# Attention and two expert layers on one core: orders of ScalarE, PE and GpSimd at three joints, and T forms by input tiles

## The reference: what is computed

```python
attn = softmax(where(mask, q @ k.T / 8, -1e9)) @ v        # -> x [1152, 512]
h = np.maximum(x @ w_in, 0.0)                             # w_in [512, 2048]
x = h * h @ w_out                                         # w_out [2048, 512]
p = domain_probs / (domain_probs.sum(-1, keepdims=True) + 1e-09)
for e in range(4):                                        # w1[e] [512, 1024], w2[e] [1024, 512]
    h = np.maximum(x @ w1[e], 0.0)
    out += p[:, e:e + 1] * (h @ w2[e])
```

## Time and profile before

| | us |
|---|---|
| median of 3 runs (641.86 to 643.49) | 642.8 |
| the profiled execution | 641.86 |
| its span, first to last instruction | 640.1 |
| PE matmuls busy | 619.5 (97%) |
| DVE busy | 375.0 |
| POOL busy | 293.8 |
| ACT busy | 247.7 |

### The profile page before, as it was taken

One profiled execution on the slowest core, in us unless ns is written; L12 is line 12 of the kernel. 1 busy time (PEld: TensorE's weight loads), 2 busy tenths in 40 slices (PEclk: granted clock), 3 DMA queues, 4 the chain that ended last, 5 costly groups with the idle time before them and its releaser, 6 DMA issues.

```text
span 640.1 us, 11296 instructions
## 1 busy us (share of the span) xinstructions
PE 619.5 (97%) x4182; PEld 576.7 (90%) x4182; DVE 375.0 (59%) x980; ACT 247.7 (39%) x674; POOL 293.8 (46%) x249
## 2 busy tenths in 40 slices
PE   8879898999999999999999999999999999999998
PEld 7769897999999999989899899899899889889986
DVE  4876557585585586673564564564565465456452
ACT  6997655362362363461151151241241331232210
POOL 4987784255055058695065064074073173260200
PEclk9999998999999999999999999999999999999999
DMA  8440301012022012021011021011021022020012
GB/s 321 158 133 2 132 2 67 1 67 67 1 67 67 2 66 68 0 67 67 1 67 67 1 67 66 2 67 67 0 67 67 1 66 67 2 67 1 0 51 98
DMA packets 16486, 35.87 MB, mean 56 GB/s; under 512 B 2864, under 2 KB 3120, under 8 KB 16432
## 3 DMA queue, kind: packets, MB, share of 16 engines
q1 hardware_dynamic: 16432, 35.15, 16.4%
HBM read 32.79 MB, written 2.36 MB: 55 GB/s over the span
## 4 chain that ended last, share of the span: by engine, by line
PE 83%; DVE 7%; ACT 6%; issue 2%; POOL 2%; DVEq 0%; ACTq 0%; POOLq 0%
PE ps L1122 27%; PE ps L1124 26%; PE ps L1123 26%; ACT prob L548 3%; DVE h_lo L873 2%; DVE ps L860 1%; PE ps L1119 1%; DVE ps L866 1%; POOL xf_lo L482 1%; DVE prob L725 1%; PE ps L1065 1%; ACT xf_hi L595 1%; PE ps L1111 1%; ACT h_hi L622 1%; ACT wa_hi L572 1%
## 5 line engine op out<-in xcount | busy, mean ns | idle before, releaser
L1122 PE MATMUL ps<-xf_hi,wa_hi 128*128 128x288 f32 x672 | 200.4, 298 | 4.1 <-ACT m L608 3.7
L1123 PE MATMUL ps<-xf_lo,wa_hi 128*128 128x288 f32 x672 | 199.2, 296 | 0.0
L1124 PE MATMUL ps<-xf_hi,wa_lo 128*128 128x288 f32 x672 | 198.6, 296 | 0.0
L448 POOL TENSOR_TENSOR wb_lo<-raw_b,wb_hi 128x512 fp32r<-128x512 f32 x48 | 60.7, 1303 | 186.6 <-ACT wb_hi L581 186.6
L1122 PEld LDWEIGHTS ps<-xf_hi,wa_hi 128*128 128x128 f32 x672 | 127.0, 189 | 5.7 <-ACT wa_hi L572 3.5
L1123 PEld LDWEIGHTS ps<-xf_lo,wa_hi 128*128 128x128 f32 x672 | 126.9, 189 | 0.5
L1124 PEld LDWEIGHTS ps<-xf_hi,wa_lo 128*128 128x128 f32 x672 | 127.3, 189 | 0.0
L1122 PE MATMUL ps<-wb_hi,h_hi 128*128 128x512 f32 x288 | 112.3, 390 | 1.1 <-DVE h_lo L876 1.1
L1124 PE MATMUL ps<-wb_hi,h_lo 128*128 128x512 f32 x288 | 112.4, 390 | 0.0
L1123 PE MATMUL ps<-wb_lo,h_hi 128*128 128x512 f32 x288 | 112.4, 390 | 0.0
L903 DVE SCALAR_TENSOR_TENSOR y<-ps,p_norm,y 128x512 f32<-128x512 f32 (+1 forms) x64 | 47.4, 742 | 96.1 <-PE ps L1124 96.1
(11 more groups left out here) (77 smaller groups left out, 868.6 us busy)
## 6 DMA issues: line engine op xcount, KB each, us to landing
raw_a<-in_wa SPq DMA_DIRECT2D x48, 256.0 KB, 3.8
raw_b<-in_wb SPq DMA_DIRECT2D x24, 512.0 KB, 4.9
q_buf<-in_q SPq DMA_DIRECT2D x8, 288.0 KB, 4.7
k_buf<-in_k SPq DMA_DIRECT2D x8, 288.0 KB, 4.6
result<-y SPq DMA_DIRECT2D x8, 256.0 KB, 2.0
v_loc<-in_v_near SPq DMA_DIRECT2D x4, 384.0 KB, 4.6
v_str<-in_v_far SPq DMA_DIRECT2D x4, 320.0 KB, 5.5
result<-y SPq DMA_DIRECT2D x2, 128.0 KB, 1.8
```

The source lines that it names most:

```text
L448: nc.gpsimd.tensor_tensor(wb_lo[:, :, cols], raw_b[:, :, cols], wb_hi[:, :, cols].bitcast(F32), ALU.subtract).then_inc(s_wb_lo, 1)
L1122: nc.tensor.matmul(dst, a_hi, b_hi, start=first, stop=False)
L1123: nc.tensor.matmul(dst, a_hi, b_lo, start=False, stop=False)
L1124: return nc.tensor.matmul(dst, a_lo, b_hi, start=False, stop=last)
```

## The change

- Attention's end, ACT: `first_product(0)` and one `x_high` come ahead of `att_out(6)`. PE: unit 1 of M2 goes behind `outputs(6)` and the transposes of pair 7.
- Block 0: the squares of C22 and C12 are made by ACT (new `squared`, activation Square) and no longer by DVE; ACT's order of h_high, y_copy and x_high is another.
- Block 2: ACT's `first_product(2)` moves up between relu and h_high of block 1's C12.
- Parts B of blocks 1 to 6: DVE takes y tile 1 between the two units of h_low (C22) and c_block (C12) of the block that went ahead.
- Experts' entry: T2, T3 and T4 of sets 2 and 3 are made in halves of one input tile each (new `half_forms`), during the parts B of blocks 6 and 7. ACT's x_high(3, ...) are spread among the h_high of block 8. POOL makes wb_low of group 4 ahead of the sums of group 5.

The diff, cut to its core:

```diff
-            return {T1: 1, T2: 2, T3: 3, T4: 4}[k]
+            return {T1: 1, T2: 5, T3: 6, T4: 7}[k]
...
-                if kind == "A" and t % 2 == 0 and 0 < t and s + 1 < SUBS:
+                if kind == "A" and t % 2 == 0 and t not in (0, BLOCKS1) and s + 1 < SUBS:
                     sums(s + 1, S1, S3, S2, S4)
                 if kind == "A" and t % 2 == 1:
                     if t > 1:
                         for d in range(KT):
                             wb_low(s, d)
-                    if t == 1:
-                        sums(1, S1, S3, S2, S4)
+                    if t in (1, BLOCKS1 + 1):
+                        sums(s + 1, S1, S3, S2, S4)
...
+            def squared(t, q):
+                for u in range(2):
+                    act.wait_ge(s_relu, tile_count(t, q, u))
+                    nc.scalar.activation(ps[:, hbank(t, q, u), 0:HT], relu[:, u, :], ACT.Square).then_inc(s_sq, 1)
...
-            att_out(NP - 2)
             first_product(0)
             x_high(0, 3)
+            att_out(NP - 2)
...
             rectified(0, C22)
+            squared(0, C22)
+            h_high(0, C22)
             y_copy(0)
             x_high(1, 1)
-            h_high(0, C22)
+            rectified(0, C12)
+            squared(0, C12)
+            h_high(0, C12)
             y_copy(1)
-            rectified(0, C12)
             x_high(1, 2)
-            y_copy(2)
-            h_high(0, C12)
-            y_copy(3)
-            for k in (3, 4, 5, 6):
-                x_high(1, k)
-                y_copy(k + 1)
+            for k in (2, 3, 4, 5):
+                y_copy(k)
+                x_high(1, k + 1)
+            y_copy(6)
+            y_copy(7)
...
+                    if t == BLOCKS1 - 1:
+                        x_high(3, 0)
                     continue
-                first_product(t)
+                if t != 2:
+                    first_product(t)
                 if t == 1:
...
+                    rectified(1, C12)
+                    first_product(2)
+                    h_high(1, C12)
                     wa_high(1, 6)
                     continue
+                if t == BLOCKS1:
+                    x_high(3, 1)
+                    x_high(3, 2)
+                    h_high(t, C11)
+                    x_high(3, 3)
+                    h_high(t, C21)
+                    x_high(3, 4)
+                    x_high(3, 5)
+                    h_high(t, C22)
+                    x_high(3, 6)
+                    h_high(t, C12)
+                    continue
...
-                if t == BLOCKS1:
-                    for k in range(FORMS):
-                        x_high(3, k)
...
+            def half_forms(i, kt):
+                c = i % 2
+                blocks, b12 = x_blocks(c)
+                dve.wait_ge(s_y, y_tiles(BLOCKS1 - 4 + i) + KT + 2 * (kt + 1))
+                for k in (T2, T3, T4):
...
+                    nc.vector.tensor_tensor(t_form[:, c, k, kt, :], a[:, kt, :], b[:, kt, :], ALU.subtract)\
+                        .then_inc(s_t[i], 1)
...
-            for u in range(2):
-                square(0, C22, u)
...
-            for u in range(2):
-                square(0, C12, u)
...
-                    if t == BLOCKS1:
-                        t_forms(3, T3, T4)
...
-                            if i == 0:
-                                for u in range(2):
-                                    h_low(follows[1], C22, u)
-                                    c_block(follows[1], C12, u)
+                            if i < 2:
+                                h_low(follows[1], C22, i)
+                                c_block(follows[1], C12, i)
...
-                        if t == BLOCKS1 - 2 and i == KT - 1:
-                            t_forms(2, T1)
-                        if t == BLOCKS1 - 1 and i == 0:
-                            t_forms(2, T3)
-                        if t == BLOCKS1 - 1 and i == 1:
-                            t_forms(2, T4)
-                        if t == BLOCKS1 - 1 and i == KT - 1:
-                            t_forms(3, T1)
-                    if t >= BLOCKS1 - 2:
-                        t_forms(t - BLOCKS1 + 4, T2)
+                        if t >= BLOCKS1 - 2 and i == KT - 1:
+                            t_forms(t - BLOCKS1 + 4, T1)
+                        if t >= BLOCKS1 - 2 and i in (KT + 1, KT + 3):
+                            half_forms(t - BLOCKS1 + 4, (i - KT) // 2)
...
-                    product(0, M2)
+                    product(0, M2, [0])
...
             prob_transposes(NP - 1, 0)
+            product(0, M2, [1])
             product(0, M6, [0])
```

More of the change, by code:

```diff
@@ L681, in _ @@
                             x_high(2, k)
+                    if t == BLOCKS1 - 1:
+                        x_high(3, 0)
                     continue
-                first_product(t)
+                if t != 2:
+                    first_product(t)
                 if t == 1:
-                    for q in (C11, C21, C22, C12):
+                    for q in (C11, C21, C22):
                         rectified(1, q)
-                        if q != C12:
-                            wa_high(1, 2 * q)
+                        wa_high(1, 2 * q)
                         h_high(1, q)
-                        if q != C12:
-                            wa_high(1, 2 * q + 1)
+                        wa_high(1, 2 * q + 1)
+                    rectified(1, C12)
+                    first_product(2)
+                    h_high(1, C12)
                     wa_high(1, 6)
+                    continue
[10 more added lines that the diff above has]
+                    h_high(t, C12)
                     continue
@@ L758, in t_forms @@
                     else:
-                        dve.wait_ge(s_y, y_tiles(BLOCKS1 - 4 + i) + (KT if k == T1 else 2 * KT))
+                        dve.wait_ge(s_y, y_tiles(BLOCKS1 - 4 + i) + KT)
                     if k == T1:
@@ L770, in t_forms @@
                     nc.vector.tensor_tensor(t_form[:, c, k, :, :], a, b, ALU.subtract).then_inc(s_t[i], 1)
+            def half_forms(i, kt):
[3 more added lines that the diff above has]
+                for k in (T2, T3, T4):
+                    if k == T2:
+                        dve.wait_ge(s_t[i], 1)
+                        a, b = blocks[B22], t_form[:, c, T1, :, :]
+                    elif k == T3:
+                        a, b = blocks[B22], b12
+                    else:
+                        dve.wait_ge(s_t[i], 3 * kt + 2)
+                        a, b = blocks[B21], t_form[:, c, T2, :, :]
+                    nc.vector.tensor_tensor(t_form[:, c, k, kt, :], a[:, kt, :], b[:, kt, :], ALU.subtract)\
+                        .then_inc(s_t[i], 1)
             def pair_t1(n):
```

## The result

| | before | changed |
|---|---|---|
| median, us | 642.33 (4 runs, 641.78 to 643.49) | 637.66 (4 runs, 637.22 to 638.49) |
| ratio | | 0.9927, 95% interval 0.9908 to 0.9946 |
| profiled execution, its span | 641.86, 640.1 | 637.22, 635.4 |

The change makes the kernel 4.7 us faster (3.5 to 5.9 by the interval), where 8.0 us was forecast. The forecast was 634.8, range 632.8 to 637.5: right way, and too low by 2.9 us. A fourth run of the kernel before (641.78) moved its median from the 642.8 that the forecast started from to 642.33.

What follows compares the result with a forecast made beforehand. TensorE's matmuls fill nearly the whole span, so only its waits could be won. Gains of 0.82 + 0.48 + 2.84 + 1.9 + 1.98 = 8.0 us off the median 642.8 gave 634.8 us, range 632.8 to 637.5.

Steps and rivals of the forecast that it cites:

- the price of the half forms: Experts' entry: three DVE halves cost 1.2 to 2.1 us; y tile slack of 1.3 covers all but 0.2 per place.
- Attention's end: Copying the first product in ScalarE's idle time removes PE's wait for it before M6: 0.82 us saved.
- Block 0: Squares on ScalarE remove the fifth output tile's 0.96 us wait but add about 0.7 at the fourth: 0.48 saved.
- Block 2: Earlier first product cuts PE's 3.15 us wait to 1.64 and the clock stays up: 2.84 us saved.
- Outputs of blocks 1 to 6: Earlier y tile removes six waits of 0.49 us, 0.18 of each coming back at tile 4: 1.9 us saved.
- Entry: Experts' entry: block 8's waits at M3 (0.64 us) and before its outputs (1.34) go: 1.98 us saved.
- (a): Block 2: the clock falls again behind the remaining 1.64 us idle, giving back 1.4: 636.2 us, chance 0.16.
- (b): Waits change place: slow Square 0.48, tile 4's wait in blocks 1 to 6 1.1, contention 0.8; 637.2 us, chance 0.12.
- (c): All edited places: the edits release nothing, since copies and forms that go first wait themselves; 642 to 643 us, chance 0.04.
- (d): Block 0: Square needs another function table, up to four loads of 1.28 us, plus clock falls; 643.2 us, chance 0.03.
- (e): More gain: block 0's squares and the outputs of blocks 1 to 6 at their good ends; 633.4 us, chance 0.03.
- parts 2 and 4: Gains from block 0's squares (0.48 us, up to 0.9) and outputs of blocks 1 to 6 (1.9, up to 2.9).

Runs made afterwards that it cites:

- third experiment: Changed kernel with set 2's half forms, and their x_high and x_low, made on 36 of 288 columns, the rest left out: 634.54 us, ratio 0.9887.
- fifth experiment: Changed kernel with block 2's first product copied at its old place, behind h_hi of C12 and the last weight copy: 639.69 us, one run.

## Why the prediction was wrong

**The step that failed** is the price of the half forms, in the paragraph on their cover. It said that three halves cost 1.2 to 2.1 us between two y tiles and PE would lose "at worst 0.2 us per place". They took 4.6, and PE lost 2.6 and then, by the clock, another 1.4 to 1.5. The cover itself was sized rightly: 4.6 - 2.6 leaves 2.0 us that PE didn't feel, so at 2.1 it would have lost about 0.1.

The earlier trace rows carried the warning. Its slow forms, 926 to 1394 ns against 752, ran beside GpSimd. I halved that time for half the columns. The third experiment shows that the surplus isn't size but the rest of GpSimd's current instruction: per instruction, up to 1.3 us. Cutting three forms into six doubled the number of times it can be paid; three of the six of set 2 paid it. Moving them also took them from behind block 6's outputs and block 7's first tiles to block 6's last tiles. GpSimd and DVE in the kernel before:

```profile
243.06 2.55 POOL L442 TENSOR_TENSOR wa_lo<-s_form,wa_hi 128x512 fp32r<-128x512 f32 x2
245.57 1.42 POOL L482 TENSOR_TENSOR xf_lo<-y,xf_hi 128x576 fp32r<-128x576 f32 x1
247.67 1.43 POOL L482 TENSOR_TENSOR xf_lo<-y,xf_hi 128x576 fp32r<-128x576 f32 x1 [0.67 <-ACT xf_hi L595]
```

```profile
246.91 0.76 DVE L770 TENSOR_TENSOR t_form<-y,t_form 128x576 f32<-128x576 f32 x1
248.37 1.34 DVE L770 TENSOR_TENSOR t_form<-y 128x576 f32<-128x576 f32 x1
250.00 0.74 DVE L770 TENSOR_TENSOR t_form<-y,t_form 128x576 f32<-128x576 f32 x1
```

There GpSimd had run out of wa_lo at 245.6, and only one of the three forms met it for more than 0.1 us, in an x_low (the one at 248.37). At block 6's last tiles wa_lo was still running. The count was in the change, and the place could have been read from these two timelines.

**The sum without that step.** 8.0 forecast, 7.65 found:

- Attention's end: 0.82 forecast, 0.86 found. The 1.6 us wait behind it stayed, as argued, and PE gained nothing there.
- Block 0: 0.48 against 0.25. Both waits were named rightly, the chain was 0.2 us longer.
- Block 2: 2.84 against 2.79, with 1.63 us of wait left and the clock at 1.00 behind it.
- Outputs of blocks 1 to 6: 1.9 against 1.6, by their matmul starts between 0.2 and 0.3 each. The y waits went, and a part came back in the next tiles, as said: at block 6 the shift goes from 6.81 us at the fourth tile to 6.64 at the sixth, with a wait of only 0.07.
- Entry: 1.98 against 2.15, with parts that aren't independent.

**The rivals.** (a), the fall of the clock in block 2, didn't happen in the profile of the changed kernel, and in the profiles of the later kernels that kept the edit the matmuls behind it start as they do there. A fall of it happened at a place that I hadn't on the list. (b), waits that change place, was the right family. Its price for contention (0.8) was a third of the 2.6 us that PE waited, and a fifth of the loss with the clock. (c) fell: the edits released 7.65 us. (d) fell: one table load, and Square at the speed of Relu. (e) fell: parts 2 and 4 came out under their forecast. **The range** ended 0.16 us too low. With the measured 4.1 in place of 0.8, (b) would have stood at 640.5, and a range above it would have held the result.

**A part that is nobody's gain.** The profiled pair differs by 1.14 us before the first edit. In the kernel before, the clock is 0.50 at 47 us, in the changed kernel 1.00 (second stretch above), with the same 2.1 us wait for probT in front. From the end of that wait to block 0's M1 the kernel before takes 5.09 us and the changed one 3.58; 0.37 of the difference is lost again because the changed kernel came to the wait later. So by the traces the change itself is worth 7.65 - 4.14 = 3.5 us, and up to 4.9 where the clock doesn't fall behind the new wait.

How often the clock falls can in part be told from its mean over a run. It is 0.995 in the profile of the kernel before, which has two falls (attention and block 2), and 0.997 in that of the changed kernel, which has one (block 7). Of the changed kernel's four runs two show 0.997 (637.22 and 637.36 us) and two 0.995 (637.97 and 638.49), as with a second fall. Of 27 further runs of the kernel before, 22 show 0.995, three 0.992 (642.9 to 643.6 us) and two 1.000 (639.17 and 639.02 us). The last two had no fall at all, so about 2.6 us of the time before, 1.4 of block 2's 2.79 among them, are the clock's and not in every run. At which place the clock fell in a run without a profile stays open.

## What to carry to other kernels

Before moving a VectorE instruction that reads two SBUF operands, look at what GpSimd does at the new place. By these runs (float32 tensor_tensor on both engines) each such instruction costs the rest of one GpSimd instruction plus at most its own time; so don't cut it into pieces there. The delay hurts only if a matmul soon wants what stands behind it on VectorE. A wait removed upstream can lengthen one downstream, so waits are priced by when their releaser is ready, not by the idle time printed.

## What the runs showed of the hardware

- VectorE, two SBUF operands, met by a running GpSimd tensor_tensor: 128x288 in 1.54 to 1.69 us instead of 0.45, 128x36 in 1.27 and 1.31 instead of 0.18. With one operand in PSUM nothing changes: y tiles 440 to 459 ns, h_lo 445 to 459. GpSimd is held up in turn: wa_lo of 128x512 lasts 1.30 us, and 1.82 beside the form at 234.22 in the changed kernel.
- The clock behind an idle PE: 0.50 after 3.15 and 3.14 us in the three profiles that have that wait, 1.00 after 1.63 and 1.85. But the two runs of the kernel before with a mean of 1.000 had no fall behind that wait either. In between it went either way: 0.50 after 2.33 in the changed kernel, 1.00 after 2.34 in the fifth experiment; after the 2.1 us in the attention 0.50 (once 0.53) in eight of the eleven profiles, those of the two kernels and the nine experiments, and 1.00 in three. Without any edit it moves this kernel by 1.3 to 1.6 us (the attention) or 1.4 us (block 7) a time.
